# Attention row sums inverted on GpSimd by a power of -1 and a Newton step, instead of by VectorE's reciprocal

## The reference

```python
def _attn_ref(q, k, v):                        # 4 x 8 heads, 576 tokens, head size 64, fp32
    scores = scale * np.matmul(q, k.transpose(0, 1, 3, 2))
    kth = np.partition(scores, -32, axis=-1)[..., -32:-31]
    scores = np.where(scores >= kth, scores, -1000000000.0)
    scores = scores - np.max(scores, axis=-1, keepdims=True)
    attn = np.exp(scores)
    attn = attn / (np.sum(attn, axis=-1, keepdims=True) + 1e-09)
    return np.matmul(attn, v)
# _moe_ref : x (2304 x 512) @ w_in (512 x 2048), relu, square, @ w_out (2048 x 512)
# _moe2_ref: 8 routed experts with a skip test, 512 -> 1024 -> 512, a gate weight for each token
```

## Time and profile before

| | |
|---|---|
| Median of 3 runs | 961.71 us (961.09 to 963.69) |
| The profiled execution | 961.93 us |
| its span in the profile | 960.1 us |
| Busy, share of the span | PE 92%, DVE 89%, POOL 72%, ACT 69% |
| Chain that ended last | PE 80%, DVE 12%, POOL 2%, ACT 2% |
| Attention ends (last `normalise`) | about 727 us |

### The profile page before, as it was taken

One profiled execution on the slowest core, in us unless ns is written; L12 is line 12 of the kernel. 1 busy time (PEld: TensorE's weight loads), 2 busy tenths in 40 slices (PEclk: granted clock), 3 DMA queues, 4 the chain that ended last, 5 costly groups with the idle time before them and its releaser, 6 DMA issues.

```text
span 960.1 us, 19356 instructions
## 1 busy us (share of the span) xinstructions
PE 882.6 (92%) x6322; PEld 721.0 (75%) x6322; DVE 854.0 (89%) x1708; ACT 661.8 (69%) x1297; POOL 694.4 (72%) x891
## 2 busy tenths in 40 slices
PE   3566799999999999999999999999999994999996
PEld 1344577888888888888888888888878983777875
DVE  6999999999999998999999999999980237888888
ACT  3677677777787677676778677777764223877875
POOL 2899798877777776787778787778785544566664
PEclk9867699999999999999999999999999995999999
DMA  8964333464354657867436544353343935555970
GB/s 317 376 215 129 118 118 120 157 203 157 115 176 167 192 162 231 241 191 240 136 119 187 169 162 162 127 187 125 132 133 126 333 117 216 200 213 184 337 279 10
DMA packets 69083, 174.76 MB, mean 182 GB/s; under 512 B 20898, under 2 KB 26018, under 8 KB 64624
## 3 DMA queue, kind: packets, MB, share of 16 engines
q1 hardware_dynamic: 67136, 168.39, 52.2%
q0 software_dynamic: 1840, 5.06, 1.6%
HBM read 153.66 MB, written 20.75 MB: 182 GB/s over the span
## 4 chain that ended last, share of the span: by engine, by line
PE 80%; DVE 12%; POOL 2%; issue 2%; ACT 2%; ACTq 0%; DMA 0%; SPq 0%; DVEq 0%; POOLq 0%
PE psum L1188 7%; PE psum L1190 7%; PE psum L1189 7%; PE psum L1128 7%; PE psum L1148 7%; PE psum L1205 7%; PE psum L1206 7%; PE psum L1207 6%; PE psum L1167 6%; DVE top L925 5%; DVE left L931 5%; PE psum L1334 2%; PE psum L1309 2%; PE psum L1131 2%; PE psum L1315 2%
## 5 line engine op out<-in xcount | busy, mean ns | idle before, releaser
L925 DVE MAX8 top<-left 128x8 f32<-128x576 f32 x432 | 305.3, 750 | 0.0
L931 DVE MATCH_REPLACE8 left<-top,left 128x576 f32<-128x576 f32 x288 | 212.1, 745 | 0.0
L565 POOL TENSOR_TENSOR s_sb<-s_sb,below 128x576 f32<-128x576 f32 x144 | 203.3, 1430 | 2.3 <-ACT below L721 2.3
L1188 PE MATMUL psum<-x_high,w_in_high 128*128 128x256 f32 x576 | 169.4, 294 | 1.6 <-POOL x_low L571 1.1
L1190 PE MATMUL psum<-x_high,w_in_low 128*128 128x256 f32 x576 | 163.8, 284 | 0.0
L1189 PE MATMUL psum<-x_low,w_in_high 128*128 128x256 f32 x576 | 163.7, 284 | 0.0
L712 ACT ACTIVATE s_sb<-psum 128x576 f32<-128x576 f32 x144 | 93.5, 650 | 88.6 <-PE psum L1128 72.5
L580 POOL TENSOR_TENSOR square<-relu 128x256 f32<-128x256 f32 x144 | 88.5, 615 | 88.2 <-ACT relu L754 87.7
L1128 PE MATMUL psum<-k_sb,q_sb 64*128 64x288 f32 x512 | 107.2, 499 | 29.6 <-ACT s_sb L712 24.4
L585 POOL TENSOR_TENSOR g_low<-square,g_high 128x256 fp32r<-128x256 f32 x144 | 107.8, 749 | 35.2 <-POOL square L580 27.0
L721 ACT ACTIVATE below<-s_sb,steep_kth 128x576 f32<-128x576 f32 x144 | 110.8, 770 | 29.8 <-POOL neg_max L553 29.8
(11 more groups left out here) (174 smaller groups left out, 1795.3 us busy)
## 6 DMA issues: line engine op xcount, KB each, us to landing
w_ring<-w_split SPq DMA_DIRECT2D x144, 512.0 KB, 4.5
weights<-w SPq DMA_DIRECT2D x32, 1024.0 KB
v_sb<-v_main SPq DMA_DIRECT2D x48, 256.0 KB, 2.6
w_split<-w_ring SPq DMA_DIRECT2D x16, 512.0 KB, 3.8
k_sb<-kT SPq DMA_DIRECT2D x32, 144.0 KB, 4.7
k_sb<-kT SPq DMA_DIRECT2D x32, 128.0 KB, 4.5
q_sb<-qT SPq DMA_DIRECT2D x32, 128.0 KB, 4.3
weights<-w_out SPq DMA_DIRECT2D x1, 4096.0 KB, 13.2
```

The costliest lines, as they stand in the source:

```text
L565: nc.gpsimd.tensor_tensor(s_sb[:, s % SBUFS, n, 0:S], s_sb[:, s % SBUFS, n, 0:S], below[:, n, :], ALU.subtract).then_inc(masked, 1)
L925: v.max(top[:, par, n, r, :], src).then_inc(topk_step, 1)
L931: v.match_replace(left[:, n, :], top[:, par, n, r, :], src, LOWEST).then_inc(topk_step, 1)
L1188: t_.matmul(dst, wh, x_high[:, j % 2, k, :], start=k == 0, stop=False)
```

## The change

The reciprocal and its wait for the exponentials leave DVE's list; what is left there is the top-32 alone. POOL gets `invert_sums(t-1)` as the last thing of turn t: four instructions on 128x2 elements, each of which waits for the one before through the semaphore sums_inverted, and a last wait on that semaphore after them. They form y = s^-1, then s*y, then s*y - 2, then (s*y - 2)*y, which is minus the refined inverse. `normalise` multiplies by that and by -1, and its own wait is gone. One small MEMSET joins the start.

```diff
+        inverse = sb("inverse", [P, 2, 2])
+        residue = sb("residue", [P, 2])
+        minus_one = sb("minus_one", [P, 2])
...
+            nc.gpsimd.memset(minus_one[:, :], -1.0).then_inc(zeros_set, 1)
+            pool.wait_ge(zeros_set, 4)
...
             def normalise(s, n):
 
-                pool.wait_ge(sums_inverted, s + 1)
                 nc.gpsimd.tensor_scalar(s_sb[:, s % SBUFS, n, 0:S], s_sb[:, s % SBUFS, n, 0:S],
-                                        sums[:, s % 2, n:n + 1], 1.0, ALU.mult, ALU.mult).then_inc(probs_done, 1)
+                                        inverse[:, s % 2, n:n + 1], -1.0, ALU.mult, ALU.mult).then_inc(probs_done, 1)
+
+            def invert_sums(s):
+
+                pool.wait_ge(exp_done, 2 * s + 2)
+                inv, now, off = inverse[:, s % 2, :], sums[:, s % 2, :], residue[:, :]
+                nc.gpsimd.tensor_tensor(inv, now, minus_one[:, :], ALU.pow).then_inc(sums_inverted, 1)
+                pool.wait_ge(sums_inverted, 4 * s + 1)
+                nc.gpsimd.tensor_tensor(off, inv, now, ALU.mult).then_inc(sums_inverted, 1)
+                pool.wait_ge(sums_inverted, 4 * s + 2)
+                nc.gpsimd.tensor_scalar(off, off, 2.0, 1.0, ALU.subtract, ALU.mult).then_inc(sums_inverted, 1)
+                pool.wait_ge(sums_inverted, 4 * s + 3)
+                nc.gpsimd.tensor_tensor(inv, off, inv, ALU.mult).then_inc(sums_inverted, 1)
+                pool.wait_ge(sums_inverted, 4 * s + 4)
...
                 for f in split_parts(t, FT):
                     split_in_low(f)
+                if 0 <= t - 1 < NS:
+                    invert_sums(t - 1)
...
-                if t >= 1:
-
-                    dve.wait_ge(exp_done, 2 * t)
-                    v.reciprocal(sums[:, (t - 1) % 2, :], sums[:, (t - 1) % 2, :]).then_inc(sums_inverted, 1)
```

More of the change, by code:

```diff
@@ L911, in _ @@
             v = nc.vector
[L913 to L931, removed]
-                if t >= 1:
-                    dve.wait_ge(exp_done, 2 * t)
-                    v.reciprocal(sums[:, (t - 1) % 2, :], sums[:, (t - 1) % 2, :]).then_inc(sums_inverted, 1)
+            for s in range(NS):
+                par = s % 2
+                dve.wait_ge(scores_copied, 2 * s + 2)
+                wait(dve, bias_set, 2 * (s - 1))
+                for r in range(ROUNDS):
+                    op = 14 * s + 4 * r
+                    for n in range(2):
+                        src = s_sb[:, s % SBUFS, n, 0:S] if r == 0 else left[:, n, :]
+                        if r:
+                            dve.wait_ge(topk_step, op + n - 1)
+                        v.max(top[:, par, n, r, :], src).then_inc(topk_step, 1)
+                    if r == ROUNDS - 1:
+                        break
+                    for n in range(2):
+                        src = s_sb[:, s % SBUFS, n, 0:S] if r == 0 else left[:, n, :]
+                        dve.wait_ge(topk_step, op + n + 1)
+                        v.match_replace(left[:, n, :], top[:, par, n, r, :], src, LOWEST).then_inc(topk_step, 1)
             chain = [0]
```

## The result

The changed kernel takes 1029.5 us (median of 4 runs, 1028.1 to 1031.2) against 962.6 for the one before: a ratio of 1.070, with a 95% interval from 1.068 to 1.072, or 67 us more. That is slower, as forecast, and inside the range, but 28 us above the predicted 1001: some 39 us more were forecast and 67 came.

A forecast was written before the change was run, and what follows sets the result against it. PE was taken to set ordinary turns at 9.38 us, with a POOL loop of 8.77 behind. Costs beyond slack, 5.0 + 5.3 + 25.6 + 4.0 + 0.4, made 40.3 us on 961.9: 1002, taken as 1001, range 984 to 1050.

The forecast's parts named there:

- a loop through POOL: Last g_low, bounds, normalisation, PE's transposes and products, ACT's relu, POOL's square, next g_low: 8.77 us a turn when unhindered.
- The two readings of the loop: Turns 10 to 13, 10.00 less L600's 1.23, and turns after the last scores: both say 8.77 us.
- What is taken away: DVE's reciprocals, 72 of 0.07 us, 5.0 in all, and two waits: counted as 0, except perhaps 0.6 us early.
- The four instructions and their hand-overs: At the turn's end on POOL before the next bounds: the power plus 0.92 us for three ordinary instructions and four hand-overs.
- p: Time of the power on POOL, with no row to show it: taken as 0.4 us, ends 0.2 and 2.3.
- d: Time the four instructions add per turn in front of the bounds: p + 0.92 = 1.32 us.
- The clock: I count nothing.: Gaps on PE could lower the granted clock; turns with L600 stayed at 1.00, so 0 us was counted.
- Slack by kind of turn: Hold-up of POOL before it costs: early 0.77, ordinary 0.61, mixed 1.23, group ends 1.64 or unbound, L600 and last turns none.
- mixed turns: Four of these take 10.00 us, with slack 1.23: 4 x 0.09 = 0.4 us expected.
- DVE as pacer: Rival: the reciprocal's place on DVE sets each turn, so 5.0 us would go: 957 us; chance 6%.
- The cheap chain: Rival: POOL's hand-overs cost nothing, d = 0.64, about 5 us more: 967 us; chance 8%.
- The long routine: Rival: the power on POOL takes 1.2 us or more; at 2.0, 146 us more, so 1108; chance 14%.

The follow-up runs named there:

- e3: The changed kernel without its Newton step, so the bare power on POOL gives the inverse: 976.8 us, ratio 1.015.
- e1: The kernel before, reciprocal and normalisation untouched, with the change's four POOL instructions added on spare tiles at each turn's end: 1024.3 us, ratio 1.065.
- e7: The changed kernel with tiles residue and minus_one declared behind the last tile, so the dense layer's tiles lie as in e1: 1022.9 us, ratio 1.064.
- e5: The changed kernel with six spare PE products before the transposes of turns 10 to 16: 1023.9 us, ratio 1.064.
- e6: The kernel before with L600 of turns 10 to 13 moved in front of the second unit's square: 960.9 us against 961.9, ratio 0.9983.
- e9: The kernel before with both the 32-byte pad of e8 and L600 moved as in e6: 959.8 us against 961.9, ratio 0.9974.
- e2: The spare chain of e1 in the kernel before, with a product in place of the power: 987.9 us, ratio 1.026.
- e8: The kernel before with an unused 32-byte tile behind sums and nothing else changed: 960.0 us against 961.9, ratio 0.9984.
- e4: The changed kernel with invert_sums in front of the square of the turn's second unit instead of at the turn's end: 982.3 us, ratio 1.021.

## Why the prediction came out as it did

- **What bounds the kernel.** Right. Ordinary turns on PE, a loop through POOL of 8.77 us behind it. The two readings of the loop (a turn with L600, and the turns at the end) gave the number that the changed kernel (10.46 - 1.68 = 8.78) and e3 (9.57 - 0.79 = 8.78) confirm.
- **What is taken away is worth nothing.** Right, by e1 against e7, to the 0.3% that their intervals leave.
- **The four instructions and their hand-overs.** The three ordinary ones and four hand-overs were put at 0.92 and measure 1.68 - 0.71 = 0.97; the TENSOR_SCALAR with a subtraction takes 0.24, not 0.20.
- **The term that was mis-sized is p.** I chose 0.4 from bounds of 0.2 and 2.3, on the thought that the fixed part of so small an instruction outweighs the power itself. It is 0.71, which is 0.51 beyond a product; only one size ran, so how much of that is fixed and how much goes by element stays open. With p = 0.71 and the 0.05 of the point above, d is 1.68 in place of 1.32. The prediction's own sum then gives 61 us in place of 40: these 0.36 are some 21 of the 28 us. The ratio between the two engines that I had cited from the Trainium skill ("GPSIMD Engine Reference", section 3.1) against the change gave 0.30 and was further off; here the power takes 4.7 times the reciprocal's 0.15. That the trace has no operation on both engines was misread: `w_low`, 128x1024, takes 2.5 to 2.9 us on POOL (L660, L666) and 1.5 to 1.6 on DVE (L1073, L1079) in the kernel before. The ratio is borne out for such a subtraction, and it doesn't carry over to a power.
- **"The clock: I count nothing."** Wrong, and the second cause of the distance: two turns of 13.2, one of 11.8 and one of 11.95 us. Filling the first few gaps gave back about 5 us (e5). My evidence was that with L600 alone the clock stayed at 1.00. But in those turns PE waited 0.35 us for the normalisation (1.34 in the first), and with L600 and the chain together it waits 2.0 to 3.8. The row was right and didn't reach that far. The first line of the earlier trace rows has a clock of 0.72 where PE is busy for 49.58 of 78 us, so a lower clock beside longer idle time was there to be seen. With d as measured the sum reaches 60.7 of the 67.1 us; the clock stands for most of the rest. Both errors go the same way: that the time still lies in the range is due to its width, and nothing cancelled.
- **Slack by kind of turn.** Right: mixed turns went from 10.00 to 10.46, the group ends of 10.41 and 11.07 moved by a few hundredths.
- **The rivals.** DVE as pacer is out for this kernel, but by little: e6 and e9, which shorten only four turns, bring it out. The cheap chain is out by e2, whose four ordinary instructions cost 1.17. The long routine was right in direction, at a third of the 2.0 us at which it was priced.

## What to carry to other kernels

Before moving an instruction to an engine with idle time, find the loop it will stand in: measure how long that loop is by itself (a turn that holds one extra instruction there, or one in which the usual pacer has less to do), and compare the slack with the instruction and its hand-overs. The same four instructions cost 67 us at one place of the turn and 20 at another. And where a change makes TensorE wait longer than the turns on which the argument rests, the granted clock of those turns is no longer evidence.

## What the runs showed of the hardware

- A power on GpSimd takes 0.71 us on 128x2 elements, a product 0.20; the difference is paid in full in the turn (0.51).
- Four small instructions on GpSimd, each waiting for the one before, take 1.17 us (e2), of which the hand-overs are 0.08 each.
- Moving the dense layer's tiles by 32 bytes made TensorE's products 3 ns shorter (283 to 280) and the kernel 0.16% faster (e8); moved by 96 bytes (an estimate, as said at e1), as the change did, they stayed at 283. On the changed kernel the step from 96 to 32 bytes was worth about 6 us, more than in the kernel before: a turn set by the loop is 0.07 to 0.08 us shorter (8.77 to 8.70, 10.46 to 10.38) and one set by TensorE 0.03. Why the loop gains more, which tile matters, and by what means, was not tried.
- Between 124 and 171 us of the changed kernel TensorE waited 3.76, 2.00, 2.00 and 2.01 us before its transposes, and its clock fell from 2.4 to 1.2 GHz for a while after the first, the second and the fourth of these waits. In e5, with spare products ahead of the transposes, the waits were 2.15, 0.38, 0.40 and 0.39, and it fell after the first alone; in e4 they were 3.50, 1.29, 1.51 and 1.51, and it was the same.
